# An attention and two-layer kernel: the preparation of the next head's q moves behind other work in each slot

## The reference

```python
scores = scale * np.matmul(q, k.transpose(0, 1, 3, 2))
...
x = (psi_rel / psi_i)[..., None]
h = np.maximum(x @ w1 + b1, 0.0)
bias = h @ w2
scores = scores + bias.transpose(2, 0, 1)[None, :, :, :]
scores = scores - np.max(scores, axis=-1, keepdims=True)
attn = np.exp(scores)
attn = attn / (np.sum(attn, axis=-1, keepdims=True) + 1e-09)
return np.matmul(attn, v).astype(np.float32)
...
h = x @ w_in
g = h - np.tanh(h)
return (g @ w_out).astype(np.float32)
...
g = x @ w_gate
silu = g * (1.0 / (1.0 + np.exp(-g)))
val = x @ w_val
return (silu * val @ w_out).astype(np.float32)
```

## Time and profile before

| | us |
|---|---|
| median of 3 runs | 1287.1 (1286.89 to 1287.58) |
| the profiled execution | 1287.1 |
| its span in the profile | 1285.3 |
| PE busy | 1202.0 (94%) |
| PEld busy | 1133.1 (88%) |
| DVE busy | 639.4 (50%) |
| ACT busy | 593.3 (46%) |
| POOL busy | 556.2 (43%) |

### The profile page before, as it was taken

One profiled execution on the slowest core, in us unless ns is written; L12 is line 12 of the kernel. 1 busy time (PEld: TensorE's weight loads), 2 busy tenths in 40 slices (PEclk: granted clock), 3 DMA queues, 4 the chain that ended last, 5 costly groups with the idle time before them and its releaser, 6 DMA issues.

```text
span 1285.3 us, 25567 instructions
## 1 busy us (share of the span) xinstructions
PE 1202.0 (94%) x8400; PEld 1133.1 (88%) x8400; DVE 639.4 (50%) x1592; ACT 593.3 (46%) x1285; POOL 556.2 (43%) x656
## 2 busy tenths in 40 slices
PE   4656689999999999999999999999999999999997
PEld 2236689999999999999999999999999999999997
DVE  8976766666666666666666653521211212112111
ACT  6876645565655655656556555521212222122211
POOL 0007757677677676776776743311111111111111
PEclk9897889999999999999999999999999999999999
DMA  6875534444344444443444434400000000000000
GB/s 179 242 233 178 159 94 126 123 130 122 111 141 123 128 123 124 127 126 108 141 124 129 125 113 166 142 25 1 25 25 27 25 23 27 1 25 1 25 1 25
DMA packets 69375, 125.02 MB, mean 97 GB/s; under 512 B 8768, under 2 KB 32320, under 8 KB 69312
## 3 DMA queue, kind: packets, MB, share of 16 engines
q1 hardware_dynamic: 69312, 124.16, 32.7%
HBM read 104.07 MB, written 20.05 MB: 97 GB/s over the span
## 4 chain that ended last, share of the span: by engine, by line
PE 48%; issue 33%; POOL 8%; DVE 7%; ACT 3%; DMA 1%; POOLq 0%; SPq 0%; DVEq 0%; ACTq 0%
PE ps_h L995 14%; PE ps_y L1012 13%; PE ps_s L950 7%; PE ps_pt L963 6%; POOL fr L513 5%; PE ps_pt L973 5%; DVE feat L733 2%; PE ps_y L973 1%; DVE wbuf L725 1%; POOL prob L479 1%; POOL fr L484 1%; DVE prob L759 1%; ACT wbuf L564 1%; DVE wbuf L774 1%; DVE wbuf L720 1%
## 5 line engine op out<-in xcount | busy, mean ns | idle before, releaser
L513 POOL TENSOR_TENSOR fr<-x_stage,fr 128x384 fp32r<-128x384 f32 x72 | 73.0, 1014 | 382.4 <-ACT fr L679 382.4
L1012 PE MATMUL ps_y<-fr,wbuf 128*128 128x288 f32 x1536 | 225.4, 295 | 1.1 <-POOL fr L484 0.4
L995 PE MATMUL ps_h<-fr,wbuf 128*128 128x288 f32 x1440 | 220.1, 296 | 0.7 <-DVE fr L801 0.7
L1012 PEld LDWEIGHTS ps_y<-fr,wbuf 128*128 128x128 f32 x1536 | 210.3, 188 | 2.9 <-POOL fr L484 2.7
L479 POOL TENSOR_SCALAR prob<-prob,rowinv 96x576 f32<-96x576 f32 x192 | 145.1, 762 | 142.1 <-DVE rowinv L769 141.4
L995 PEld LDWEIGHTS ps_h<-fr,wbuf 128*128 128x128 f32 x1440 | 201.1, 189 | 1.6 <-issue 0.9
L774 DVE TENSOR_TENSOR wbuf<-ps_pt,wbuf 128x480 fp32r<-128x480 f32 x176 | 115.8, 658 | 166.2 <-ACT wbuf L564 165.5
L564 ACT ACTIVATE wbuf<-ps_pt 128x480 fp32r<-128x480 f32 x176 | 100.7, 572 | 199.8 <-PE ps_pt L963 199.4
L1094 PE MATMUL ps_y<-wbuf,fr 128*128 128x512 f32 x648 | 162.5, 395 | 1.3 <-POOL fr L513 1.3
L556 ACT ACTIVATE prob<-prob,negmax 96x576 f32<-96x576 f32 x192 | 147.8, 770 | 5.9 <-DVE negmax L759 5.4
L484 POOL TENSOR_TENSOR fr<-g_b,fr 128x288 fp32r<-128x288 f32 x128 | 112.4, 878 | 81.3 <-ACT fr L574 81.3
(11 more groups left out here) (107 smaller groups left out, 1829.5 us busy)
## 6 DMA issues: line engine op xcount, KB each, us to landing
biasb<-bias_scratch SPq DMA_DIRECT2D x192, 216.0 KB, 3.9
k_raw<-k_t SPq DMA_DIRECT2D x63, 288.0 KB, 2.8
v_raw<-v_p SPq DMA_DIRECT2D x64, 160.0 KB, 3.4
q_raw<-q_t SPq DMA_DIRECT2D x64, 144.0 KB, 2.5
biasb<-w_chunks SPq DMA_DIRECT2D x32, 256.0 KB, 3.7
prob<-w_chunks SPq DMA_DIRECT2D x8, 768.0 KB, 4.3
bias_scratch<-x_stage SPq DMA_DIRECT2D x36, 144.0 KB, 2.6
bias_scratch<-y_stage SPq DMA_DIRECT2D x36, 144.0 KB, 2.6
```

What stands on the lines that cost most here:

```text
L513: eng.tensor_tensor(a_lo[c % 2], a_b, a_hi[c % 2].bitcast(F32), ALU.subtract).then_inc(p_alo, 1)
L995: mm = eng.matmul(hidden_bank(u, c)[:, 0:T1], w[:, cols], x[:, d, :], start=d == 0 and i == 0, stop=d == KC - 1 and i == 2)
L1012: mm = eng.matmul(ps_y[:, d, 0:T1], w[:, cols], g[c % 2], start=c == 0 and i == 0, stop=c == C1 - 1 and i == 2)
```

## The change

Two functions `slot` are reordered, ScalarE's and VectorE's. No instruction is added, removed or resized, and no wait is added or taken away; the slots of attention alone are not touched, nor are the orders of TensorE, GpSimd and the transfers.

- ScalarE, joint slots except s = 7: `q_high` stood before `exp_tile(2)` and now stands behind `o_part` and the second `tanh`, before `g_high`. In the slots with s = 7 it stays where it was.
- VectorE, all joint slots: `inverse(1)` stood behind `score(2)` and now stands before it. `q_low` stood before `x_out` and now stands behind the second `gated`, in the slots with s = 7 too.

```diff
@@ ScalarE, slot @@
                 if late:
                     tanh(m + 1, hidden_bank(moe[0], 1))
-                if prep:
-                    q_high(n + 1, 1 - par, moe)
+                    if prep:
+                        q_high(n + 1, 1 - par, moe)
                 if qk:
                     exp_tile(n, par, 2)
...
                     o_part(n - 1, 1 - par, o_bank)
                 if not late:
                     tanh(m + 1, hidden_bank(moe[0], 1))
+                    if prep:
+                        q_high(n + 1, 1 - par, moe)
                     g_high(m + 1, 1)
@@ VectorE, slot @@
                 if qk:
+                    inverse(n, par, 1)
                     score(n, par, 2, moe)
-                    inverse(n, par, 1)
-                if prep:
-                    q_low(n + 1, 1 - par, moe)
                 if pv and not last:
                     x_out(n - 1, 1 - par, o_bank, x_chunk)
                 w2_lows(w2_splits[0])
                 gated(m + 1, 1, hidden_bank(moe[0], 1))
+                if prep:
+                    q_low(n + 1, 1 - par, moe)
                 if qk and not last:
                     inverse(n, par, 2)
```

## The result

The changed kernel takes 1323.15 us (median of 4 runs, 1322.73 to 1324.02), the kernel before 1286.99 us (median of 4 runs beside it). The ratio of the two is 1.0284, with a 95% interval of 1.0266 to 1.0302: the change makes the kernel slower by 36 us, where 32 were forecast (1319.3). The span of the profiled execution grew from 1285.3 to 1320.6 us.

The account below looks back on a forecast made before the run. TensorE was taken to bound the joint stage, busy 554.5 of 560 us, with later `q_low` delaying it. 41 x 0.70 + 7 x 0.50 + 6 x 0 = 32.2 us on 1287.1 gave 1319.3 us; 8-in-10 range 1297 to 1325.

Parts of the forecast that it names:

- main term: Ordinary joint slots: TensorE's load starts 0.70 us later in each of 41 slots, 28.7 us in all.
- main case: Whole kernel: 32.2 us slower, 1319.3 us, own range 1314 to 1323; chance 0.74.
- a second loss later in the slot: Joint slots: TensorE would have to lose again later in the slot for more than 1323 us; chance 0.01.
- Steps 1 to 3: Ordinary slot, ScalarE and VectorE: third exponential starts at 412.20, `gated` at 413.98, `q_low` at 414.47.
- the bound with the hold: VectorE: `q_low`, starting at row 64, waits until `gated` has finished, so starts 0.49 after it; otherwise 0.37.
- Step 4: Ordinary slot, GpSimd: `norm(1)` comes at 414.36, 0.21 earlier than now, and takes 0.74, to 415.10.
- Step 5: Ordinary slot: `norm(1)` leads by 0.11 and `q_low` stands still meanwhile, ending 0.31 after it, at 415.41.
- `q_low` gets through first: Rival, ordinary slots: `q_low` asks before `norm(1)`, losing 0.22 a slot, 1299.6 us (1294.7 without the hold); chance 0.17.
- step 6: Ordinary slot: TensorE's load follows `q_low`'s end by 0.12, at 415.53 instead of 414.83, losing 0.70 us.
- shared bandwidth: Alternative to exclusion of `q_low` and `norm(1)`: 0.53 us lost an ordinary slot, sum 25.2 us instead of 32.2.
- First and last slots: A unit's first slot loses 0.50 us; its last loses 0, with a gain of up to 0.38 as other bound.
- Faster: Rival, units' ends and first slots: cast and `x_out` come earlier, up to 4.3 us gained, 1282.8 us; chance 0.04.

Follow-up runs that it names:

- run 4: Changed kernel with `norm(1)` on GpSimd also waiting for the next head's `q_low`, so that `q_low` is first: 1304.03 us, ratio 1.0136.
- run 1: Kernel before with only `inverse(1)` put ahead of `score(2)` on VectorE: 1285.78 us, ratio 0.9994.
- run 2: Changed kernel with `score(2)` ahead of `inverse(1)` again on VectorE, the rest as changed: 1295.00 us, ratio 1.0062.
- run 5: Changed kernel with TensorE's scores waiting for `v_score` first and `v_q` last: 1319.05 us, ratio 1.0252.
- run 3: Changed kernel with ScalarE's order undone, `q_high` ahead of the third exponential again: 1324.46 us, ratio 1.0293.
- runs 7 to 9: Kernel before, s = 7: `o_part`, `x_out` earlier, 1287.85 us; plus `norm(1)` waiting for x's low parts, 1286.87; plus g's split between the norms, 1285.53.

## Why the prediction was right

The sum's main term was right, and for its reason. The forecast was too small: without the first joint slot, which lies outside the joint part, it makes 31.7 us there against 36.9 measured, 5.2 us less. The time, 1323.15, lies just above the range that the prediction gave its main case (1314 to 1323). What the prediction had named for such a time, a second loss later in the slot, did not occur: from the load to the second exponential's read it is 6.51 us, and was 6.49. TensorE's new waits are 46 (48 forecast).

- *Steps 1 to 3, when `q_low` starts.* Counted from the second exponential's read (424.70), the third exponential came after 1.46 (1.39 forecast), `q_low` after 3.72 (3.66). It started 0.49 after `gated` (427.93 to 428.42), the bound with the hold, and so it did in all 54 slots; `inverse`, which starts at row 0, follows `gated` by 0.37. Without the hold `q_low` would have come at 428.30, only 0.04 behind `norm(1)`, nearer than any lead of GpSimd that a run shows.
- *Step 4, GpSimd.* `norm(1)` after 3.56 (3.55 forecast), the k split 0.68. `norm(1)`'s lead was 0.16 and, in the slots of the other parity, 0.21; forecast was 0.11.
- *Step 5, the exclusion.* `q_low` ended 0.31 after `norm(1)`, 4.61 after the read (4.60 forecast). Run 4 shows the hold by itself: with the order turned round, 19 us come back. So the hold is about half of the loss, and the late place of `q_low` the other. The prediction had this split in its bounds (0.22 a slot if `q_low` got through first, of 0.70), with the short latency of step 6. That it is all or nothing, and no shared bandwidth, shows in runs 1 and 2, where whoever came first kept its own duration (k split 0.68 and 1.45). The prediction counted three cases in the trace of the kernel before. There were more: the ordinary slot's `q_low` took 0.64 because `split_g` had the path until 412.23, and it ended 0.31 after that:

```profile
411.42 0.81 POOL L484 TENSOR_TENSOR fr<-g_b,fr 128x288 fp32r<-128x288 f32 x1 [0.78 <-ACT fr L574]
```

- *Step 6, the mis-sized term.* From `q_low`'s end to the load I took 0.12, from the first head, whose code is written out. In the loop slots it was 0.23, in the written-out ones 0.07. An ordinary slot lost 0.83 and 0.67 instead of 0.70: +4.7 us in 36 loop slots, -0.2 in 5 written-out ones. A unit's first slots add 0.6 and its last ones 0.1, which gives the 5.2 us. In a loop slot 0.11 of the 0.13 us is this latency. Run 5 halved it by the order of waits alone.
- *First and last slots.* 0.6 lost (0.50 forecast) with the same latency behind it, and 0.02 (0 forecast). The hope for a gain in the last slot failed at the k split, as said.
- *The rivals.* "`q_low` gets through first" did not happen here, but it was near. In the written-out slots the lead of `norm(1)` was down to 0.06 us. The changed kernel and run 5 each have two such slots; here is one of each:

```profile
748.49 0.74 POOL L479 TENSOR_SCALAR prob<-prob,rowinv 96x576 f32<-96x576 f32 x1
...
748.55 0.99 DVE L751 SCALAR_TENSOR_TENSOR fr<-q_raw,fr 64x288 fp32r<-64x288 f32 x1
```

```profile
746.64 1.84 POOL L479 TENSOR_SCALAR prob<-prob,rowinv 96x576 f32<-96x576 f32 x2
...
746.70 0.46 DVE L751 SCALAR_TENSOR_TENSOR fr<-q_raw,fr 64x288 fp32r<-64x288 f32 x1
```

  With the same lead the changed kernel's `q_low` waited (0.99, as in the two such slots of run 3), and that of run 5 did not (0.46), while its two norms took 1.84 instead of 1.47. A lead of 0.06 us is thus near the edge, but only run 5 shows VectorE winning there: in all 36 ordinary loop slots of run 1 GpSimd was ahead by 0.06 to 0.07 and won, and from 0.11 on I saw only GpSimd win. My estimated lead was 0.11, on the right side by little: an error of 0.1 us in a sum of five or six terms would have given the other outcome.
- *Faster.* Nothing of it showed; runs 7 to 9 say what it would have needed.

What stays open: which part of the 0.07 to 0.23 us is the register work behind a wait and which the wait itself. Only the order was changed, not the number of waits.

## What to carry to other kernels

When work moves later on one engine, check what runs then on the engine that it shares a path with, to a tenth of a microsecond; slack against the consumer alone is not enough. Costs of parts of a reordering do not add: two moves at 0 and 8 us were 37 together. About a third of the surplus came because one move had used up the slack and the other then counted in full; the rest because together they put another instruction first on the shared path. To tell the two apart, force the order with one added wait, as in run 4. Where an instruction in a loop waits for several semaphores, try to wait last for the one that comes last: it gave 0.11 us a slot here, but cost 0.05 where the code was written out.

## What the runs showed of the hardware

- A VectorE instruction with two inputs in SBUF and a GpSimd one that reads SBUF exclude each other. `q_low` takes 0.46 us alone; behind a GpSimd instruction it ends 0.30 to 0.31 us after that one's end, or 0.46 us after its own start, if that is later (0.34 us after GpSimd's end in a unit's first slot of run 3). One that waits is served as the other ends, ahead of a GpSimd instruction that comes after it (run 2). `x_out` and `gated`, which read one input from PSUM, took their 0.45 to 0.46 us beside the k split as well (changed kernel: `gated` from 427.93, the k split until 428.29). The Trainium skill ("SBUF — State Buffer", section "Who interferes with whom") states the exclusion; how close a race can be is from these runs: GpSimd ahead by 0.06 to 0.07 us won in 40 slots and lost in 2 (run 5), VectorE ahead by 0.02 to 0.03 won (run 1).
- TensorE's load follows the instruction that it waits for by 0.23 us in a loop slot with another wait behind this one, and by 0.12 with it as the last (changed kernel and run 5). In the written-out slots it was 0.07 and 0.12.
